# A two-layer gated network on one core: the fifth pass of the first product as pairs of 64-row matmuls

## The chip, the cores and the metric

The kernel runs on one NeuronCore of a Trainium2 chip. The metric is the device time of one execution in microseconds (us), lower is better. The time before is 1227.66 us, the median of three runs that lie between 1227.56 and 1228.3 us.

## The reference, cut to what matters

```python
# x: (2, 4096, 192), weight: (8 heads, 7 taps)
w   = softmax(weight, axis=-1)
out = causal 7-tap convolution of x along the sequence, one set of taps per head
x   = out.reshape(8192, 192)
h   = x @ moe_w_in                     # 192 -> 2048
x   = (h * clip(h + 3, 0, 6) / 6) @ moe_w_out      # 2048 -> 192
h   = x @ moe2_w_in                    # 192 -> 2048
g   = where(h > 0, h, exp(min(h, 0)) - 1)
out = g @ moe2_w_out                   # 2048 -> 192
```

All data are float32.

## The kernel before, in words

**Tiles.** The 8192 tokens are cut into 16 tiles of 512. A tile lies transposed, features on the partitions, 512 tokens along the free axis. The 192 features are split into part a (128 partitions) and part b (64 partitions). The 2048 hidden features are 16 chunks of 128. Two chunks make a group (`CPG` = 2), so a layer of a tile has eight groups (`GROUPS`), and the whole run has 16 x 2 x 8 = 256 groups.

**Precision.** TensorE works in float32r. To keep accuracy each operand is split into a high part (rounded to float32r) and a low part (the rest), and hi x hi, lo x hi and hi x lo are summed in PSUM.

**First product.** `chunk_product` computes a chunk of h. Five matmuls, each of 128 rows by 128 columns of weights and 512 moving columns, accumulate into one PSUM bank: for part a `win_hi_a` x `in_hi_a`, `win_lo_a` x `in_hi_a`, `win_hi_a` x `in_lo_a`; for part b `win_hi_b` x `in_b` and `win_lo_b` x `in_b`. `in_b` holds the high part of the 64 features of b in partitions 0 to 63 and their low part in 64 to 127; the `win_*_b` tiles hold the 64 rows of b twice. So the fourth matmul gives hi x hi and hi x lo in one pass. The fifth gives lo x hi, the wanted term, and lo x lo, which isn't needed. `first_product` does this for the two chunks of a group and adds 1 to `h_ready`.

**Second product.** `second_product` takes the gated values of a group (`g_hi`, `g_lo`) through ten matmuls of the same shape into the accumulators `acc_a` and `acc_b`.

**Order on TensorE.** `phase` is one layer of one tile: for each group g the first product of g and then the second product of g - 2 (`LAG` = 2); the two before that belong to the phase ahead. So TensorE's program is ten matmuls of a first product, ten of a second, in turn, 5120 in all. `pair` orders the phases: layer 1 of tile i, then layer 2 of tile i - 1.

**PSUM.** Eight banks: `h_ps[0]` and `h_ps[1]`, two banks each, by the parity of the group; two for `acc_a` and two for `acc_b`. The first product of group G may begin when group G - 2 has been read (`g_ready` at least G - 1).

**Other engines.** After `h_ready` ScalarE reads `h_ps` into `hidden` (L274 relu for layer 1, L276 exp for layer 2), VectorE combines it with `h_ps` (L404, or L407 and L409) and adds to `g_ready`, ScalarE makes `g_hi` (L284), VectorE `g_lo` (L413). Between these VectorE computes the convolution of a later tile (L355, L357). The input of the next layer is made in `take_mlp1` and `take_mlp1_b`, that of layer 1 in `split_conv`: ScalarE writes the high part (L246, L247, L254, L259), VectorE the low part (L374, L376, L383, L389). GpSimd makes low weights in the first stretch alone; SyncE issues the loads and stores.

Of the kernel before, what the change touches and what calls it, by code (L numbers as in the profile page):

```python
# [29 lines left out]
F32R = mybir.dt.float32r  # L30
# [7 lines left out]
P = 128  # L38
DA = P
DB = D - P  # L40
TOK = 512
# [3 lines left out]
CPG = 2  # L45
# [3 lines left out]
PIECES = 4  # L49
# [3 lines left out]
SIXTH = 1.0 / 6.0  # L53


def build(nc, x_win, tap_w, w_in1, w_out1, w_in2, w_out2, out_t):
    w_in, w_out = (w_in1, w_in2), (w_out1, w_out2)
    with ExitStack() as ctx:
        def sb(name, shape, dt=F32):
            return ctx.enter_context(nc.sbuf_tensor(name, shape, dt))  # L60

        def ps(name, shape):
            return ctx.enter_context(nc.psum_tensor(name, shape, F32))

        def sem(name):
            return ctx.enter_context(nc.semaphore(name))
# [4 lines left out]
        win_hi_b = [sb(f"win_hi_b{m}", [P, FF], F32R) for m in range(2)]  # L71
        win_lo_b = [sb(f"win_lo_b{m}", [P, FF], F32R) for m in range(2)]
# [10 lines left out]
        conv_b = sb("conv_b", [DB, TOK])  # L83
# [4 lines left out]
        in_hi_a = [sb(f"in_hi_a{m}", [DA, TOK], F32R) for m in range(2)]  # L88
        in_lo_a = [sb(f"in_lo_a{m}", [DA, TOK], F32R) for m in range(2)]
        in_b = [sb(f"in_b{m}", [2 * DB, TOK], F32R) for m in range(2)]  # L90

        hidden = sb("hidden", [P, 2, CPG * TOK])
        g_hi = sb("g_hi", [P, PARTS, CPG * TOK], F32R)
# [3 lines left out]
        sum_b1 = sb("sum_b1", [DB, TOK])  # L97
# [5 lines left out]
        h_ps = [ps(f"h_ps{s}", [P, CPG * TOK]) for s in range(2)]  # L103
# [8 lines left out]
        w_split = sem("w_split")  # L112
# [4 lines left out]
        conv_hi = sem("conv_hi")  # L117
        in1_ready = sem("in1_ready")
        in2_ready = sem("in2_ready")
        h_ready = sem("h_ready")  # L120
        act_done = sem("act_done")
        expm1_done = sem("expm1_done")
        g_ready = sem("g_ready")
# [3 lines left out]
        take1 = sem("take1")  # L127
# [16 lines left out]
        def end1(i):  # L144


            return GROUPS if isinstance(i, int) and i == 0 else first_group1(i) + GROUPS
# [88 lines left out]
        def _(act):  # L236
# [5 lines left out]
            def split_conv(t, dst, reused):  # L242
                act.wait_ge(tap_done, 2 * TAPS * t + 2 * TAPS)
                if reused:
                    act.wait_ge(h_ready, end1(t - 1))
                nc.scalar.copy(in_hi_a[dst][:, :], conv_a[:, :]).then_inc(conv_hi, 1)  # L246
                nc.scalar.copy(in_b[dst][0:DB, :], conv_b[:, :]).then_inc(conv_hi, 1)  # L247

            def take_mlp1(t, acc, dst, input_read):

                act.wait_ge(parts_used, end1(t))
                if input_read is not None:
                    act.wait_ge(h_ready, input_read)
                nc.scalar.mul(in_hi_a[dst][:, :], acc_a[acc][:, :], SIXTH).then_inc(take1, 1)  # L254
                nc.scalar.copy(half_b1[:, :], acc_b[acc][DB:2 * DB, :]).then_inc(take1, 1)

            def take_mlp1_b(t, dst):
                act.wait_ge(take1_b, t + 1)
                nc.scalar.mul(in_b[dst][0:DB, :], sum_b1[:, :], SIXTH).then_inc(take1, 1)  # L259

            def take_mlp2(t, acc):
                act.wait_ge(parts_used, end2(t))
                act.wait_ge(stored, 32 * (t + 1))
                nc.scalar.copy(half_b2[:, :], acc_b[acc][DB:2 * DB, :]).then_inc(take2, 1)
                nc.scalar.copy(out_a[:, :], acc_a[acc][:, :]).then_inc(take2, 1)
# [27 lines left out]
            high_weights(2)  # L293
            act.wait_ge(tap_done, 2 * TAPS)
            nc.scalar.copy(in_b[1][0:DB, :], conv_b[:, :]).then_inc(conv_hi, 1)
            act.wait_ge(three_set, 1)

            for g in range(GROUPS):
                nonlinear(0, 0, g)
                if g == TAPS - 1:  # L300
                    split_conv(1, 0, False)
                high_part(0, g)
                if g + 3 < 2 * PIECES:
                    high_weights(g + 3)
# [45 lines left out]
        def _(dve):  # L350
# [19 lines left out]
                    tap(part, k)  # L370

            def split_conv(t, dst):
                dve.wait_ge(conv_hi, 2 * t + 2)
                nc.vector.tensor_tensor(in_lo_a[dst][:, :], conv_a[:, :], in_hi_a[dst][:, :].bitcast(F32),  # L374
                                        ALU.subtract).then_inc(in1_ready, 1)
                nc.vector.tensor_tensor(in_b[dst][DB:2 * DB, :], conv_b[:, :], in_b[dst][0:DB, :].bitcast(F32),  # L376
                                        ALU.subtract).then_inc(in1_ready, 1)

            def take_mlp1(t, acc, dst):
                dve.wait_ge(take1, 3 * t + 2)  # L380
                nc.vector.tensor_tensor(sum_b1[:, :], acc_b[acc][0:DB, :], half_b1[:, :],
                                        ALU.add).then_inc(take1_b, 1)
                nc.vector.scalar_tensor_tensor(out=in_lo_a[dst][:, :], in0=acc_a[acc][:, :], scalar=SIXTH,  # L383
                                               in1=in_hi_a[dst][:, :].bitcast(F32), op0=ALU.mult,
                                               op1=ALU.subtract).then_inc(in2_ready, 1)

            def take_mlp1_b(t, dst):
                dve.wait_ge(take1, 3 * t + 3)
                nc.vector.scalar_tensor_tensor(out=in_b[dst][DB:2 * DB, :], in0=sum_b1[:, :], scalar=SIXTH,  # L389
                                               in1=in_b[dst][0:DB, :].bitcast(F32), op0=ALU.mult,  # L390
                                               op1=ALU.subtract).then_inc(in2_ready, 1)
# [46 lines left out]
            for part in range(2):  # L438
                for k in range(TAPS):
# [3 lines left out]
                    if part == 1 and k == 1:  # L443
                        dve.wait_ge(conv_hi, 1)
                        nc.vector.tensor_tensor(in_lo_a[1][:, :], conv_a[:, :], in_hi_a[1][:, :].bitcast(F32),  # L445
                                                ALU.subtract).then_inc(in1_ready, 1)
            dve.wait_ge(conv_hi, 2)
            nc.vector.tensor_tensor(in_b[1][DB:2 * DB, :], conv_b[:, :], in_b[1][0:DB, :].bitcast(F32),  # L448
                                    ALU.subtract).then_inc(in1_ready, 1)

            for g in range(GROUPS):
                nonlinear(0, 0, g)
                if g < TAPS - 1:
                    conv_tap(1, g)
                    if g == TAPS - 2:
                        conv_tap(1, TAPS - 1)
                if g == TAPS - 1:
                    split_conv(1, 0)
                low_part(0, g)
# [42 lines left out]

        @block.tensor
        def _(pe):
            def chunk_product(m, g, c, src, a=True, b=True):

                f = slice((g * CPG + c) * P, (g * CPG + c + 1) * P)
                dst = h_ps[g % 2][:, c * TOK:(c + 1) * TOK]
                passes = []
                if a:  # L510
                    passes += [(win_hi_a, in_hi_a), (win_lo_a, in_hi_a), (win_hi_a, in_lo_a)]
                if b:
                    passes += [(win_hi_b, in_b), (win_lo_b, in_b)]
                for n, (w, x) in enumerate(passes):
                    mm = nc.tensor.matmul(dst, w[m][:, f], x[src][:, :], start=(a and n == 0),  # L515
                                          stop=(b and n == len(passes) - 1))
                return mm

            def first_product(m, base, g, src, load=False):

                G = base + g
                if load and g % 2 == 0:
                    pe.wait_ge(w_split, 2 * (2 * PIECES * m + g) + 2)
                if not (isinstance(G, int) and G < 2):
                    pe.wait_ge(g_ready, G - 1)
                for c in range(CPG):
                    mm = chunk_product(m, g, c, src)
                mm.then_inc(h_ready, 1)

            def second_product(m, base, g, acc, load=False):  # L530

# [19 lines left out]
            def first_start():  # L551

                pe.wait_ge(in1_ready, 1)
                pe.wait_ge(w_split, 1)
                for g in range(2):
                    for c in range(CPG):
                        chunk_product(0, g, c, 1, b=False)
                pe.wait_ge(in1_ready, 2)
                pe.wait_ge(w_split, 2)
                for g in range(2):  # L560
                    for c in range(CPG):
                        mm = chunk_product(0, g, c, 1, a=False)
                    mm.then_inc(h_ready, 1)

            def phase(m, base, src, before, acc, ready, acc_free, load=False):


                ready()
                for g in range(GROUPS):
                    if before is not None or g >= 2:  # L570
                        first_product(m, base, g, src, load)
                    if g < LAG:
                        if before is not None:
                            before(GROUPS - LAG + g)
                    else:
                        if g == LAG:
                            acc_free()
                        second_product(m, base, g - LAG, acc, load)
# [68 lines left out]
```

## Time and profile before

| | value |
|---|---|
| median of 3 runs | 1227.66 us (1227.56 to 1228.3) |
| profiled execution, its span | 1227.6 us |
| PE (matmuls) busy | 1205.1 us, 98% |
| PEld (weight loads) busy | 967.4 us, 79% |
| DVE (VectorE) busy | 920.2 us, 75% |
| ACT (ScalarE) busy | 620.2 us, 51% |
| POOL (GpSimd) busy | 53.9 us, 4% |
| mean granted TensorE clock | 0.996 |

The profile lists each instruction of an engine with its start and its duration. Matmuls are pipelined: a record goes from the read of the first column to the modelled end, and the next record begins before it. So the cost of a matmul in a dense stream is the distance from start to start, and its record's length says how long the engine needs to run empty. The only time given for the profiled execution is its span, from the first to the last instruction; it agrees with the median of the runs within 0.1 us, so the two are taken as one.

### The profile page before, as it was taken

What the parts mean: (1) busy time and instruction counts of PE and PEld (TensorE: products, weight loads), DVE (VectorE), ACT (ScalarE), POOL (GpSimd) and SP (SyncE); (2) the same over time, 40 slices, a digit from 0 to 9 for tenths busy, and PEclk for the clock granted to TensorE, in tenths of its full rate; (3) what the DMA queues carried; (4) which work ended last, traced back from release to release, by engine and by line L of the source; (5) the groups of instructions that cost most, each with busy time, mean ns of one, the idle gap of its engine ahead of it and who ended that gap; (6) DMA issues with size and microseconds to landing.
All of it is one profiled execution on the core that took longest, in us unless ns stands there. A gap on an engine that the chain in (4) does not pass through costs nothing.

```text
span 1227.6 us, 13953 instructions
## 1 busy us (share of the span) xinstructions
PE 1205.1 (98%) x5120; PEld 967.4 (79%) x5120; DVE 920.2 (75%) x969; ACT 620.2 (51%) x658; POOL 53.9 (4%) x36
## 2 busy tenths in 40 slices
PE   4999999999999999999999999999999999999998
PEld 2888888888888888888888888888888888888886
DVE  7888786877777777777777867778687777776665
ACT  3674555545555454554545545455544555545444
POOL 3472000000000000000000000000000000000000
PEclk8999999999999999999999999999999999999999
DMA  4220000000000000000000000000000000000000
GB/s 133 86 61 14 1 26 0 0 26 0 26 0 21 4 0 26 0 26 0 0 26 0 26 0 0 26 0 26 0 0 26 0 26 0 9 5 5 9 1 26
DMA packets 13727, 20.21 MB, mean 16 GB/s; under 512 B 1424, under 2 KB 5520, under 8 KB 13712
## 3 DMA queue, kind: packets, MB, share of 16 engines
q1 hardware_dynamic: 13568, 20.00, 5.3%
q8 instruction: 10, 0.16, 0.1%
q14 instruction: 5, 0.04, 0.0%
q10 hardware_dynamic: 144, 0.01, 0.0%
HBM read 13.71 MB, written 6.29 MB: 16 GB/s over the span
## 4 chain that ended last, share of the span: by engine, by line
PE 98%; DVE 1%; DMA 0%; ACT 0%; issue 0%; SPq 0%; DVEq 0%; ACTq 0%
PE h_ps L515 49%; PE acc_b L548 10%; PE acc_b L541 10%; PE acc_a L547 10%; PE acc_a L539 10%; PE acc_a L540 10%; DVE conv_b L357 1%; DVE conv_a L357 0%; DMA xwin_b<-x_win 0%; DVE conv_b L355 0%; DVE hidden L404 0%; DVE in_lo_a L445 0%; ACT hidden L274 0%; DVE in_b L448 0%; DVE out_b L396 0%
## 5 line engine op out<-in xcount | busy, mean ns | idle before, releaser
L284 ACT CAST g_hi<-hidden 128x1024 fp32r<-128x1024 f32 x256 | 269.2, 1051 | 371.6 <-DVE hidden L409 244.4
L413 DVE TENSOR_TENSOR g_lo<-hidden,g_hi 128x1024 fp32r<-128x1024 f32 x256 | 313.2, 1223 | 128.0 <-ACT g_hi L284 127.5
L404 DVE SCALAR_TENSOR_TENSOR hidden<-hidden,h_ps 128x1024 f32<-128x1024 f32 x128 | 156.2, 1221 | 111.3 <-ACT hidden L274 111.2
L515 PE MATMUL h_ps<-in_hi_a,win_hi_a 128*128 128x512 f32 x512 | 204.7, 400 | 16.5 <-DVE in_lo_a L445 15.4
L274 ACT ACTIVATE hidden<-h_ps,three 128x1024 f32<-128x1024 f32 x128 | 142.9, 1117 | 131.9 <-PE h_ps L515 131.9
L515 PE MATMUL h_ps<-in_b,win_hi_b 128*128 128x512 f32 x512 | 203.8, 398 | 1.8 <-DVE in_b L448 1.8
L515 PE MATMUL h_ps<-in_hi_a,win_lo_a 128*128 128x512 f32 x512 | 204.4, 399 | 0.0
L515 PE MATMUL h_ps<-in_lo_a,win_hi_a 128*128 128x512 f32 x512 | 204.2, 399 | 0.0
L515 PE MATMUL h_ps<-in_b,win_lo_b 128*128 128x512 f32 x512 | 203.8, 398 | 0.0
L541 PE MATMUL acc_b<-g_hi,wout_b 128*128 128x512 f32 x512 | 203.0, 396 | 0.0
L548 PE MATMUL acc_b<-g_lo,wout_b 128*128 128x512 f32 x512 | 203.0, 396 | 0.0
L547 PE MATMUL acc_a<-g_lo,wout_hi_a 128*128 128x512 f32 x512 | 203.0, 396 | 0.0
L539 PE MATMUL acc_a<-g_hi,wout_hi_a 128*128 128x512 f32 x512 | 203.0, 396 | 0.0
L540 PE MATMUL acc_a<-g_hi,wout_lo_a 128*128 128x512 f32 x512 | 203.0, 396 | 0.0
L276 ACT ACTIVATE hidden<-h_ps 128x1024 f32<-128x1024 f32 x128 | 131.7, 1029 | 80.8 <-PE h_ps L515 80.8
L409 DVE TENSOR_TENSOR hidden<-hidden,h_ps 128x1024 f32<-128x1024 f32 x128 | 156.3, 1221 | 4.4
L515 PEld LDWEIGHTS h_ps<-in_hi_a,win_hi_a 128*128 128x128 f32 x512 | 97.2, 190 | 40.8 <-DVE in_lo_a L445 15.4
L407 DVE TENSOR_SCALAR hidden<-hidden 128x1024 f32<-128x1024 f32 x128 | 89.9, 703 | 52.5 <-ACT hidden L276 51.3
L515 PEld LDWEIGHTS h_ps<-in_b,win_hi_b 128*128 128x128 f32 x512 | 96.8, 189 | 25.9 <-DVE in_b L448 2.3
L515 PEld LDWEIGHTS h_ps<-in_lo_a,win_hi_a 128*128 128x128 f32 x512 | 97.3, 190 | 23.8
L515 PEld LDWEIGHTS h_ps<-in_hi_a,win_lo_a 128*128 128x128 f32 x512 | 97.3, 190 | 23.6
L515 PEld LDWEIGHTS h_ps<-in_b,win_lo_b 128*128 128x128 f32 x512 | 96.9, 189 | 23.6
(47 smaller groups left out, 857.8 us busy)
## 6 DMA issues: line engine op xcount, KB each, us to landing
xwin_a<-x_win SPq DMA_DIRECT2D x16, 259.0 KB, 2.8
raw_in<-w_in SPq DMA_DIRECT2D x8, 512.0 KB, 4.7
out_t<-out_a SPq DMA_DIRECT2D x16, 256.0 KB, 2.6
raw_out<-w_out SPq DMA_DIRECT2D x8, 384.0 KB, 3.6
xwin_b<-x_win SPq DMA_DIRECT2D x16, 129.5 KB, 3.0
out_t<-out_b SPq DMA_DIRECT2D x16, 128.0 KB, 2.3
taps<-tap_w ACTq DMA_DIRECT2D x1, 7.0 KB, 2.3
```

Of the source, the lines that this page charges most:

```text
L274: ins = nc.scalar.activation(hidden[:, g % 2, :], h_ps[g % 2][:, :], ACT.Relu, bias=three[:, 0:1])
L276: ins = nc.scalar.activation(hidden[:, g % 2, :], h_ps[g % 2][:, :], ACT.Exp)
L284: nc.scalar.copy(g_hi[:, g % PARTS, :], hidden[:, g % 2, :]).then_inc(hi_ready, 1)
L404: nc.vector.scalar_tensor_tensor(out=v, in0=v, scalar=6.0, in1=h_ps[g % 2][:, :], op0=ALU.min, op1=ALU.mult).then_inc(g_ready, 1)
L409: nc.vector.tensor_tensor(v, v, h_ps[g % 2][:, :], ALU.max).then_inc(g_ready, 1)
L413: nc.vector.tensor_tensor(g_lo[:, g % PARTS, :], hidden[:, g % 2, :], g_hi[:, g % PARTS, :].bitcast(F32), ALU.subtract).then_inc(lo_ready, 1)
L515: mm = nc.tensor.matmul(dst, w[m][:, f], x[src][:, :], start=(a and n == 0), stop=(b and n == len(passes) - 1))
L539: nc.tensor.matmul(acc_a[acc][:, :], wout_hi_a[m][:, f, :], x, start=first, stop=False)
L540: nc.tensor.matmul(acc_a[acc][:, :], wout_lo_a[m][:, f, :], x, start=False, stop=False)
L541: nc.tensor.matmul(acc_b[acc][:, :], wout_b[m][:, f, :], x, start=first, stop=False)
L547: nc.tensor.matmul(acc_a[acc][:, :], wout_hi_a[m][:, f, :], x, start=False, stop=end)
L548: mm = nc.tensor.matmul(acc_b[acc][:, :], wout_b[m][:, f, :], x, start=False, stop=end)
```

## The change

The fifth matmul of each chunk (`win_lo_b` x `in_b`, 128 rows) is taken out. In its place stands a matmul of 64 rows that computes only lo x hi. For the first chunk of a group it uses partitions 0 to 63, the upper half of the array, for the second chunk partitions 64 to 127, the lower half. The lower half needs the high part of b on partitions 64 to 127, so a second input tile `in_b2` gets it there, by one more ScalarE instruction in each place where `in_b` is written.

The four halves of two successive groups are issued together, in the even group's `first_product`: eight full matmuls of group g, its two halves (they end the sum of group g), the wait for the banks of group g + 1, and the two halves of g + 1 (they begin its sum). In the odd group's `first_product` eight full matmuls remain, and no wait. `first_start` does the same at the very beginning, with both groups' halves at the end. The counts that VectorE waits for (`conv_hi`, `take1`) rise, since each is now added to once more.

```diff
+        in_b2 = [sb(f"in_b2{m}", [2 * DB, TOK], F32R) for m in range(2)]
...
                 nc.scalar.copy(in_b[dst][0:DB, :], conv_b[:, :]).then_inc(conv_hi, 1)
+                nc.scalar.copy(in_b2[dst][DB:2 * DB, :], conv_b[:, :]).then_inc(conv_hi, 1)
...
                 nc.scalar.mul(in_b[dst][0:DB, :], sum_b1[:, :], SIXTH).then_inc(take1, 1)
+                nc.scalar.mul(in_b2[dst][DB:2 * DB, :], sum_b1[:, :], SIXTH).then_inc(take1, 1)
...
             nc.scalar.copy(in_b[1][0:DB, :], conv_b[:, :]).then_inc(conv_hi, 1)
+            nc.scalar.copy(in_b2[1][DB:2 * DB, :], conv_b[:, :]).then_inc(conv_hi, 1)
...
-                dve.wait_ge(conv_hi, 2 * t + 2)
+                dve.wait_ge(conv_hi, 3 * t + 3)
...
-                dve.wait_ge(take1, 3 * t + 3)
+                dve.wait_ge(take1, 4 * t + 4)
...
-                    passes += [(win_hi_b, in_b), (win_lo_b, in_b)]
+                    passes += [(win_hi_b, in_b)]
                 for n, (w, x) in enumerate(passes):
-                    mm = nc.tensor.matmul(dst, w[m][:, f], x[src][:, :], start=(a and n == 0),
-                                          stop=(b and n == len(passes) - 1))
+                    mm = nc.tensor.matmul(dst, w[m][:, f], x[src][:, :], start=(first and n == 0),
+                                          stop=(last and n == len(passes) - 1))
                 return mm
...
+            def half_products(m, g, src, first):
+
+                for c in range(CPG):
+                    rows = slice(c * DB, (c + 1) * DB)
+                    f = slice((g * CPG + c) * P, (g * CPG + c + 1) * P)
+                    mm = nc.tensor.matmul(h_ps[g % 2][:, c * TOK:(c + 1) * TOK], win_lo_b[m][rows, f],
+                                          (in_b, in_b2)[c][src][rows, :], start=first, stop=not first)
+                return mm
+
+            def bank_free(G):
                 if not (isinstance(G, int) and G < 2):
                     pe.wait_ge(g_ready, G - 1)
-                for c in range(CPG):
-                    mm = chunk_product(m, g, c, src)
-                mm.then_inc(h_ready, 1)
+
+            def first_product(m, base, g, src, load=False):
+
+                G = base + g
+                if g % 2 == 0:
+                    if load:
+                        pe.wait_ge(w_split, 2 * (2 * PIECES * m + g) + 2)
+                    bank_free(G)
+                    for c in range(CPG):
+                        chunk_product(m, g, c, src)
+                    half_products(m, g, src, False).then_inc(h_ready, 1)
+                    bank_free(G + 1)
+                    half_products(m, g + 1, src, True)
+                else:
+                    for c in range(CPG):
+                        mm = chunk_product(m, g, c, src, first=False, last=True)
+                    mm.then_inc(h_ready, 1)
...
                 for g in range(2):
                     for c in range(CPG):
-                        mm = chunk_product(0, g, c, 1, a=False)
-                    mm.then_inc(h_ready, 1)
+                        chunk_product(0, g, c, 1, a=False, first=False)
+                for g in range(2):
+                    half_products(0, g, 1, False).then_inc(h_ready, 1)
```

## Rows read from the trace of the kernel before

**Rows 1.** The page: busy time of each engine; the chain that ended last.

```profile
PE 1205.1 (98%) x5120; PEld 967.4 (79%) x5120; DVE 920.2 (75%) x969; ACT 620.2 (51%) x658; POOL 53.9 (4%) x36
...
PE 98%; DVE 1%; DMA 0%; ACT 0%; issue 0%; SPq 0%; DVEq 0%; ACTq 0%
```

**Rows 2.** Waits, whole run: who waited for whom, total us, times, longest.

```profile
PE h_ps L515 <- DVE in_lo_a L445: 15.4, 1, 15.4
...
PE h_ps L515 <- DVE in_b L448: 1.8, 1, 1.8
...
PE h_ps L515 <- DVE hidden L404: 1.1, 1, 1.1
```

**Rows 3.** One tile's length in the middle: busy time, count, granted clock.

```profile
300.00:375.00 75.00, 75.00 (x322) 60.30 (x321) 56.63 (x61) 37.77 (x39) 0.00 (x0) 1.00 0.04 11
```

**Rows 4.** Timeline, layer 1: end of one first product, start of the next.

```profile
602.07 0.39 PE L515 MATMUL h_ps<-in_b,win_lo_b 128*128 128x512 f32 x1
602.07 0.19 PEld L539 LDWEIGHTS acc_a<-g_hi,wout_hi_a 128*128 128x128 f32 x1
602.30 0.40 PE L539 MATMUL acc_a<-g_hi,wout_hi_a 128*128 128x512 f32 x1
...
602.50 1.12 ACT L274 ACTIVATE hidden<-h_ps,three 128x1024 f32<-128x1024 f32 x1 [1.23 <-PE h_ps L515]
...
603.65 1.22 DVE L404 SCALAR_TENSOR_TENSOR hidden<-hidden,h_ps 128x1024 f32<-128x1024 f32 x1 [1.01 <-ACT hidden L274]
...
604.64 0.40 PE L515 MATMUL h_ps<-in_hi_a,win_hi_a 128*128 128x512 f32 x1
```

**Rows 5.** Timeline of PE at the start: a restart from empty, full clock.

```profile
22.46 0.50 PE L515 MATMUL h_ps<-in_b,win_hi_b 128*128 128x512 f32 x1 [1.77 <-DVE in_b L448]
22.80 0.40 PE L515 MATMUL h_ps<-in_b,win_lo_b 128*128 128x512 f32 x1
```

**Rows 6.** Timeline of PEld at the same restart: the two weight loads.

```profile
22.46 0.19 PEld L515 LDWEIGHTS h_ps<-in_b,win_hi_b 128*128 128x128 f32 x1 [2.31 <-DVE in_b L448]
22.57 0.19 PEld L515 LDWEIGHTS h_ps<-in_b,win_lo_b 128*128 128x128 f32 x1
```

**Rows 7.** Timeline, layer 2: PE, and VectorE's reading of the bank.

```profile
564.58 0.40 PE L515 MATMUL h_ps<-in_b,win_lo_b 128*128 128x512 f32 x1
...
569.27 0.39 PE L515 MATMUL h_ps<-in_b,win_lo_b 128*128 128x512 f32 x1
...
566.80 1.22 DVE L409 TENSOR_TENSOR hidden<-hidden,h_ps 128x1024 f32<-128x1024 f32 x1
```

**Rows 8.** Groups of instructions, whole run: busy us, mean ns of one.

```profile
L276 ACT ACTIVATE hidden<-h_ps 128x1024 f32<-128x1024 f32 x128 | 131.7, 1029 | 80.8 <-PE h_ps L515 80.8
L407 DVE TENSOR_SCALAR hidden<-hidden 128x1024 f32<-128x1024 f32 x128 | 89.9, 703 | 52.5 <-ACT hidden L276 51.3
L259 ACT ACTIVATE in_b<-sum_b 64x512 fp32r<-64x512 f32 x16 | 9.9, 616 | 0.0
L247 ACT CAST in_b<-conv_b 64x512 fp32r<-64x512 f32 x15 | 9.3, 617 | 0.0
```

**Rows 9.** Timelines of ACT, PE and DVE in the first 31 us.

```profile
21.07 0.62 ACT L295 CAST in_b<-conv_b 64x512 fp32r<-64x512 f32 x1 [8.26 <-DVE conv_b L357]
...
23.27 0.39 PE L515 MATMUL h_ps<-in_b,win_lo_b 128*128 128x512 f32 x1
...
24.91 1.22 DVE L404 SCALAR_TENSOR_TENSOR hidden<-hidden,h_ps 128x1024 f32<-128x1024 f32 x1 [2.51 <-ACT hidden L274]
...
26.28 0.76 PE L515 MATMUL h_ps<-in_hi_a,win_hi_a 128*128 128x512 f32 x1 [1.11 <-DVE hidden L404]
26.84 0.63 PE L515 MATMUL h_ps<-in_hi_a,win_lo_a 128*128 128x512 f32 x1
...
30.25 0.56 PE L515 MATMUL h_ps<-in_b,win_lo_b 128*128 128x512 f32 x1
...
29.09 1.22 DVE L404 SCALAR_TENSOR_TENSOR hidden<-hidden,h_ps 128x1024 f32<-128x1024 f32 x1 [0.62 <-ACT hidden L274]
```

More of the change, by code:

```diff
@@ L379, in take_mlp1 @@
             def take_mlp1(t, acc, dst):
-                dve.wait_ge(take1, 3 * t + 2)
+                dve.wait_ge(take1, 4 * t + 2)
                 nc.vector.tensor_tensor(sum_b1[:, :], acc_b[acc][0:DB, :], half_b1[:, :],
@@ L446, in _ @@
                                                 ALU.subtract).then_inc(in1_ready, 1)
-            dve.wait_ge(conv_hi, 2)
+            dve.wait_ge(conv_hi, 3)
             nc.vector.tensor_tensor(in_b[1][DB:2 * DB, :], conv_b[:, :], in_b[1][0:DB, :].bitcast(F32),
@@ L504, in _, with chunk_product @@
         def _(pe):
-            def chunk_product(m, g, c, src, a=True, b=True):
+            def chunk_product(m, g, c, src, a=True, b=True, first=True, last=False):
                 f = slice((g * CPG + c) * P, (g * CPG + c + 1) * P)
@@ L512, in chunk_product @@
                 if b:
-                    passes += [(win_hi_b, in_b), (win_lo_b, in_b)]
+                    passes += [(win_hi_b, in_b)]
                 for n, (w, x) in enumerate(passes):
-                    mm = nc.tensor.matmul(dst, w[m][:, f], x[src][:, :], start=(a and n == 0),
-                                          stop=(b and n == len(passes) - 1))
-                return mm
+                    mm = nc.tensor.matmul(dst, w[m][:, f], x[src][:, :], start=(first and n == 0),
+                                          stop=(last and n == len(passes) - 1))
+                return mm
+            def half_products(m, g, src, first):
[6 more added lines that the diff above has]
+            def bank_free(G):
+                if not (isinstance(G, int) and G < 2):
+                    pe.wait_ge(g_ready, G - 1)
             def first_product(m, base, g, src, load=False):
                 G = base + g
[L522 to L525, printed above, removed]
-                for c in range(CPG):
-                    mm = chunk_product(m, g, c, src)
-                mm.then_inc(h_ready, 1)
+                if g % 2 == 0:
[11 more added lines that the diff above has]
+                    mm.then_inc(h_ready, 1)
             def second_product(m, base, g, acc, load=False):
```

## The prediction

> **What bounds the kernel now.** I read the busy times and the chain first: TensorE's matmuls are busy for 1205.1 of 1227.6 us, and 98% of the chain that ended last lies on PE [rows 1]. The table of waits says the same from the other side. PE waited for another engine three times in the whole run, 15.4, 1.8 and 1.1 us, all in the first 27 us [rows 2]. A stretch of 75 us from the middle is filled to the end at a granted clock of 1.00 [rows 3]. So everywhere but in the first 27 us the time is the number of places in TensorE's stream times the length of a place.
>
> A place is the distance from start to start. From 602.07 to 604.64 there are eleven places, 2.57 / 11 = 0.234 us [rows 4]. The last matmuls of two successive first products stand twenty places apart, 564.58 and 569.27, which gives 4.69 / 20 = 0.234 [rows 7]. I use 0.234. A record is 0.40 long, so a matmul is on its way for about 0.16 us more after its successor has started. The reader is to see two things there: the weight load of the next matmul begins when the current one begins (both at 602.07 [rows 4]), so it is covered; and the change from the first product to the second, or from bank to bank, costs nothing.
>
> VectorE, with 56.63 of 75 us, and ScalarE, with 37.77, have room [rows 3].
>
> **What is saved if all goes well.** 256 groups are 128 pairs of groups. A pair had four fifth passes, four places. It now has four halves; if the two of a group run beside each other they need two places. That is 2 x 0.234 = 0.468 us per pair, 128 x 0.468 = 59.9 us in all. The number of instructions doesn't change (5120 matmuls, 5120 weight loads); all of the gain hangs on the overlap.
>
> **What the change of height costs.** The stream was uniform: every matmul uses all 128 rows. Now it changes twice per pair, full to half and back, 256 times in all. No row shows a matmul of 64 rows or such a change, so its price has to be bounded.
>
> Lower bound: nothing. The weights of the half load while the last full matmul runs, as they do today, and the change costs 0.
>
> Upper bound: the array has to be empty before weights can go into it in another division. Then three things stand in a row: the last matmul runs out, 0.397 us from its start (0.40 in the record, 0.396 as the mean of one; ScalarE, which reads its bank, starts 0.43 after it, 602.07 to 602.50, so the record's length is about right [rows 4]); the load; the next matmul. The price of a load that nothing covers is in the restart at 22.46: the first load starts at 22.46 and the second at 22.57; the matmul behind starts at 22.80, 0.34 after the first instead of 0.234, so 0.107 us are open [rows 5, 6]. A change then takes 0.397 + 0.107 = 0.504 from start to start instead of 0.234, an extra 0.270 us.
>
> Which value? The nearest row is the restart from empty, the only place at full clock where a load isn't ahead. The load that runs ahead in the stream today goes into an array that is divided as the running matmul is; for a load that divides it otherwise, I have no row that shows it can be ahead. I take the upper one, without great confidence, and keep 0 for the range.
>
> The Trainium skill's TensorEngine Tiling page (Key Properties) states that changing the tiling mode, as opposed to the tile, drains the TensorE. No row before shows it. By it the sum is the one that I take; without it, the sum would be that of the rival with free changes.
>
> **The block, in order.** Time 0 is the start of the last full matmul. It has run out at 0.397. The load of the upper half ends at 0.504, and its matmul starts; the load of the lower half follows at 0.611, and its matmul starts beside the first. The second upper half is one place behind the first, 0.738. The second lower half starts at 0.611 + 0.234 = 0.845. It has run out at 1.242, and the next full matmul starts after its load at 1.349. Before, the same two full matmuls stood five places apart, 1.171. So a pair becomes 0.178 us longer: 128 x 0.178 = 22.8 us slower. Break-even is near: if the array counts as empty 0.308 us after a start, instead of 0.397, the block costs what it did.
>
> **The wait moved ahead.** The halves of g + 1 write the banks of group g - 1, so `g_ready` of g - 1 is asked for ten places earlier than before, behind the first set of halves. In layer 2, the slower, group g - 1 ends at 564.58 and VectorE has read it at 566.80 + 1.22 = 568.02. The tenth matmul of the next first product, about where the wait will stand, starts at 569.27 [rows 7]. That leaves 1.25 us. In layer 1 VectorE ends at 603.65 + 1.22 = 604.87 and the tenth place is at 604.64 + 9 x 0.234 = 606.75, 1.88 us later [rows 4]. So it is met and I cost it at nothing. If it were late, the second product behind it would be late with it, and all other engines.
>
> **The added ScalarE work.** One more instruction of 0.616 us per write of `in_b`, 32 in all [rows 8]. In `take_mlp1_b` two of them (1.23) stand beside VectorE's L404 of 1.22 us [rows 4]; VectorE waits for them after it. In `split_conv` three stand behind the exp, about 1.85, beside L407 and L409 (0.703 + 1.22 = 1.92), which `high_part` waits for anyway [rows 4, 8]. Both are covered to within 0.1 us, and that is inside the 1.25 us above. Were the cover gone, 0.62 once per layer of a tile would make at most 32 x 0.62 = 20 us, but only after the 1.25 us are used up. GpSimd, SyncE and every DMA keep their work and their order.
>
> **The start.** There PE does wait. The added copy stands behind L295 (21.07, 0.62 long) and ahead of VectorE's last low part: about 0.52 us later, since such copies overlap by a tenth [rows 9]. `h_ready` of group 0 came with the matmul at 23.27; now it comes with the lower half, 0.397 + 0.107 + 0.107 = 0.61 behind the same place. The chain to 26.28, where PE waits for L404, gets 1.1 us longer [rows 9]. Behind it the moved wait bites once: L404 of group 1 ends at 29.09 + 1.22 = 30.31, and the tenth matmul starts at 30.25 [rows 9]. I add 0.4 for it: 1.5 us in all.
>
> **Sum.** 1227.6 + 22.8 + 1.5 = 1251.9, so 1252 us. The span and the median of the runs are the same within 0.1 us.
>
> **The rivals.**
>
> Changes free or nearly so (the other side). The mechanism is one: weights of the other height load ahead, under the running matmul. Then a pair saves 0.468, or 0.361 if the lower half stays behind by its load of 0.107. 1227.6 - 59.9 + 1.5 = 1169, or 1227.6 - 46.2 + 1.5 = 1183 us. For it: all of today's loads are ahead, whatever tile they feed, and nothing in a row says height matters. It decides from the point where a change costs less than 0.18 us (half of 0.361).
>
> The load open, but the next one able to stream in without waiting for the tail. Then the 0.397 in the block becomes 0.234: the block is 0.234 + 0.107 + 0.341 + 0.234 + 0.107 = 1.023 instead of 1.171, 128 x 0.148 = 18.9 us saved, 1210 us. For it: today a new matmul starts 0.16 us before the last has run out. The emptying and the load need not both be exposed.
>
> The halves don't overlap, so that the change doesn't do what it says. Then four halves take four places. With free changes nothing is won: 1229 us. With emptying: 0.397 + 0.107 + 3 x 0.234 + 0.397 + 0.107 = 1.710, 0.539 more per pair, 1227.6 + 69.0 + 1.5 = 1298 us. Against it: the two halves share no rows, no bank and no input tile. The Trainium skill's page TensorE: Matmul & The Clock Gate (Part 3, Measured speedup vs the span model) gives 3.07 times for four row tiles of 32 rows, so it has them overlap. No row before shows this.
>
> TensorE's clock. It fell once in the run, behind idle times of 1 us and more [rows 2, 9]; there a place was 0.43 (26.84 after a first one at 26.28 that had an open load). The new gaps are 0.27 us. A fall for a tenth of the run would cost about 100 us; I give it almost nothing.
>
> **How the numbers follow.** Emptying at each change, halves side by side: 0.46, forecast 1252, own range 1242 (emptying in 0.36) to 1261 (0.43). Open load without emptying: 0.22, near 1210. Free changes: 0.16, 1169 to 1183. No overlap with emptying: 0.07, 1298. No overlap, free changes: 0.05, 1229. The remaining 0.04 is spread above. The range 1176 to 1264 leaves out the lower half of the free case, the 1298 and the tails. Within 0.2% of before, 2.5 us, is about what a measurement here can tell from no change. The case at 1229 and the crossings of the 0.22 and 0.46 cases near break-even give 0.07. Faster: 0.40. Slower: 0.53.
>
> **What the profile after would show.** The last full matmul to the first upper half: 0.50 by my forecast, 0.34 by the open load, 0.234 if free. The same back to full height. Upper to lower half 0.107, against 0.234 if they don't overlap. PE's waits still only in the first 30 us. VectorE's and ScalarE's idle times larger. I am wrong if weight loads of the new height start together with the last full matmul.

## The result, and the profile after

The changed kernel takes 1222.6 us (median of 4 runs, 1222.41 to 1223.79) against 1227.7 us before; the ratio is 0.9961 with a 95% interval of 0.9949 to 0.9972. It is faster by 0.4%, 5.1 us. The forecast was 1252 us, slower by 2%.

Ahead of the prediction the span of the profiled execution before (1227.6 us) and the median of the runs were taken as one. They aren't: every run that has both shows a device time 1.8 us longer than its span. So the profiled execution before is about 1.8 us slower than the median run, at a mean granted clock of 0.996, where nineteen later runs of that kernel have 0.998 to 1.000. Below, spans are set beside spans and medians beside medians.

The page of the changed kernel, busy times and the chain that ended last, answers to [rows 1]:

```profile
PE 1196.2 (98%) x5120; PEld 899.4 (74%) x5120; DVE 918.1 (75%) x969; ACT 640.5 (52%) x690; POOL 52.4 (4%) x36
...
PE 97%; DVE 2%; ACT 0%; DMA 0%; issue 0%; ACTq 0%
PE h_ps L519 39%; PE acc_a L562 12%; PE acc_b L564 10%; PE acc_a L570 10%; PE acc_b L571 10%; PE acc_a L563 10%; PE h_ps L528 7%; DVE conv_a L361 1%; DVE conv_b L361 0%; DVE hidden L408 0%; DMA taps<-tap_w 0%; ACT hidden L277 0%; DVE in_lo_a L449 0%; DVE conv_b L359 0%; ACT g_hi L287 0%
```

TensorE is still the bound, with the same 5120 matmuls. L528 is the new half product. One group of L528 shows the engine at work; this is the timeline of PE in layer 1, where [rows 4] stood before:

```profile
600.89 0.40 PE L519 MATMUL h_ps<-in_b,win_hi_b 128*128 128x512 f32 x1
601.22 0.74 PE L528 MATMUL h_ps<-in_b,win_lo_b 64*128 64x512 f32 x4
601.89 0.50 PE L562 MATMUL acc_a<-g_hi,wout_hi_a 128*128 128x512 f32 x1
602.23 0.40 PE L563 MATMUL acc_a<-g_hi,wout_lo_a 128*128 128x512 f32 x1
```

And the weight loads of the same stretch:

```profile
600.66 0.19 PEld L519 LDWEIGHTS h_ps<-in_b,win_hi_b 128*128 128x128 f32 x1
601.22 0.30 PEld L528 LDWEIGHTS h_ps<-in_b,win_lo_b 64*128 64x128 f32 x4 [0.37 <-issue]
601.89 0.19 PEld L562 LDWEIGHTS acc_a<-g_hi,wout_hi_a 128*128 128x128 f32 x1 [0.37 <-issue]
602.00 0.19 PEld L563 LDWEIGHTS acc_a<-g_hi,wout_lo_a 128*128 128x128 f32 x1
```

Four things are to be seen.

- The first load of a half comes 0.33 us behind the start of the last full matmul (600.89 to 601.22). In the stream a load starts with the matmul ahead of it. So the change of height does make the engine wait, and 0.33 is longer than a place (0.234) and shorter than a matmul's record (0.40). In this block it is 0.326; over all blocks after the first 45 us it is 0.318 to 0.327, on average 0.322.
- Four loads of 0.19 us each fit into 0.30 us: two start together (0.004 us apart in the trace), and two more 0.11 behind them. The lower half's load does not queue behind that of the upper half.
- The four halves end 0.74 after 601.22, at 601.96. The last of them are 0.39 long, so the second pair starts at 601.57, one place and one load (0.34) behind the first.
- From 601.57 to 601.89 the engine empties again (0.32), and L562 has an open load: 0.50 long instead of 0.40, and its successor comes after 0.34 us.

The block, from the last full matmul to the place where the next one streams, is 0.326 + 0.107 + 0.234 + 0.326 + 0.107 = 1.100 us here, on average 1.097. Five places were 1.171. The stream as a whole says the same: the 4640 matmuls behind the 200th (116 pairs of groups) take 1087.08 us before and 1078.41 after, 0.075 us less per pair.

The waits answer to [rows 2] (who waited for whom, total us, times, longest):

```profile
PEld h_ps L528 <- issue: 47.8, 128, 0.7
...
PEld acc_a L562 <- issue: 46.4, 126, 0.4
...
PE h_ps L519 <- DVE in_lo_a L449: 16.2, 1, 16.2
...
PE h_ps L519 <- DVE hidden L408: 2.2, 1, 2.2
PE h_ps L519 <- DVE in_b L452: 2.2, 1, 2.2
...
PE h_ps L528 <- DVE hidden L408: 0.8, 1, 0.8
```

The two "issue" rows are new, one for each direction of the change, once in (nearly) every block. "Issue" means that the load waited for nothing that the profile shows, no other engine and no DMA. The moved wait shows once (0.8 us, at the start), and nowhere else.

The start lost more than forecast. Timeline of PE in the changed kernel, first 40 us:

```profile
16.22 0.80 PE L519 MATMUL h_ps<-in_hi_a,win_hi_a 128*128 128x512 f32 x1 [16.22 <-DVE in_lo_a L449]
...
25.00 1.22 PE L528 MATMUL h_ps<-in_b,win_lo_b 64*128 64x512 f32 x4
28.41 0.47 PE L519 MATMUL h_ps<-in_hi_a,win_hi_a 128*128 128x512 f32 x1 [2.20 <-DVE hidden L408]
...
32.50 0.80 PE L528 MATMUL h_ps<-in_b,win_lo_b 64*128 64x512 f32 x2 [0.84 <-DVE hidden L408]
33.23 0.80 PE L562 MATMUL acc_a<-g_hi,wout_hi_a 128*128 128x512 f32 x1
33.82 0.63 PE L563 MATMUL acc_a<-g_hi,wout_lo_a 128*128 128x512 f32 x1
...
39.12 0.40 PE L562 MATMUL acc_a<-g_hi,wout_hi_a 128*128 128x512 f32 x1
```

The same matmul as the last of these, in the kernel before:

```profile
35.34 0.39 PE L539 MATMUL acc_a<-g_hi,wout_hi_a 128*128 128x512 f32 x1
```

It is 3.8 us later. 0.8 of that is there already at the first matmul (15.38 before); nothing of the change lies ahead of it, and in the traces of the ten kernels shown here that matmul stands anywhere between 15.17 and 17.47. The other 3.0 us are the later `h_ready` of group 0, the wait of 0.84 at 32.50, and the clock: behind idle time the engine ran at the lower of its two levels (1.2 and 2.4 GHz), where the record at 33.82 is 0.63 long instead of 0.40. The kernel before had such a stretch too, of about 7 us against about 10 us here. At that level a place is 0.43 instead of 0.234 us, so the 3 us more cost at most about 1.5 us, by my estimate; no run takes the clock and the later signals apart.

The account closes: 128 x 0.075 = 9.6 us saved, 3.8 us lost, 5.8 us. The two spans, 1227.6 and 1222.0, differ by 5.6, the medians by 5.1.

### The profile page after: what moved, and what is told of

The parts are those of the page before. It is cut to its first block, busy times and chain, and to the rows that moved or that the text cites. A ratio compares the mean times of both kernels' runs of the same rounds, so it can differ in the third digit from the quotient of the medians.

```text
span 1222.0 us, 13985 instructions
## 1 busy us (share of the span) xinstructions
PE 1196.2 (98%) x5120; PEld 899.4 (74%) x5120; DVE 918.1 (75%) x969; ACT 640.5 (52%) x690; POOL 52.4 (4%) x36
## 4 chain that ended last, share of the span: by engine, by line
PE 97%; DVE 2%; ACT 0%; DMA 0%; issue 0%; ACTq 0%
PE h_ps L519 39%; PE acc_a L562 12%; PE acc_b L564 10%; PE acc_a L570 10%; PE acc_b L571 10%; PE acc_a L563 10%; PE h_ps L528 7%; DVE conv_a L361 1%; DVE conv_b L361 0%; DVE hidden L408 0%; DMA taps<-tap_w 0%; ACT hidden L277 0%; DVE in_lo_a L449 0%; DVE conv_b L359 0%; ACT g_hi L287 0%
## 5 line engine op out<-in xcount | busy, mean ns | idle before, releaser
L562 PE MATMUL acc_a<-g_hi,wout_hi_a 128*128 128x512 f32 x512 | 216.5, 423 | 0.0
L562 PEld LDWEIGHTS acc_a<-g_hi,wout_hi_a 128*128 128x128 f32 x512 | 96.6, 189 | 64.6 <-issue 46.4
L571 PEld LDWEIGHTS acc_b<-g_lo,wout_b 128*128 128x128 f32 x512 | 96.5, 189 | 23.6
```

What stands on the lines that cost most here:

```text
L562: nc.tensor.matmul(acc_a[acc][:, :], wout_hi_a[m][:, f, :], x, start=first, stop=False)
L571: mm = nc.tensor.matmul(acc_b[acc][:, :], wout_b[m][:, f, :], x, start=False, stop=end)
```

## The experiments

**All halves in the upper half of the array**

```diff
-                    rows = slice(c * DB, (c + 1) * DB)
+                    rows = slice(0, DB)
...
-                                          (in_b, in_b2)[c][src][rows, :], start=first, stop=not first)
+                                          in_b[src][rows, :], start=first, stop=not first)
```

> All four halves use partitions 0 to 63 (in_b), so no two can run beside each other; the changes of height stay. Theory A (the two halves of a group overlap fully, each change of height waits until the array has run out, 0.326 us from the last start, and then 0.107 for an open load): the block, from the last full matmul to the next full one, goes from 1.100 to 0.326 + 0.107 + 3 x 0.234 + 0.326 + 0.107 = 1.568 us; 128 x 0.468 = 59.9 more than the 1222.6 of the changed kernel, about 1282 us. Theory B (halves did not overlap, and the gain came from somewhere else, such as shorter records): no change, about 1222 us.

Measured: 1279.78 us, ratio 1.0421 (1.0404 to 1.0439). Timeline of PE:

```profile
607.73 0.39 PE L519 MATMUL h_ps<-in_b,win_hi_b 128*128 128x512 f32 x1
608.05 1.19 PE L528 MATMUL h_ps<-in_b,win_lo_b 64*128 64x512 f32 x4
609.17 0.50 PE L562 MATMUL acc_a<-g_hi,wout_hi_a 128*128 128x512 f32 x1
609.51 0.40 PE L563 MATMUL acc_a<-g_hi,wout_lo_a 128*128 128x512 f32 x1
```

The four take 1.19 us instead of 0.74, two places more; the gaps on both sides stay (607.73 to 608.05, and an open load in L562). The overlap of upper and lower half is real and is worth 57.2 us here. Within one height the next load is ahead again, since the added halves cost a place each and no load. All four read `in_b` here and the gaps stay, so the reading of the second tile `in_b2` doesn't make them.

**Full matmuls in the same places**

```diff
-                    rows = slice(c * DB, (c + 1) * DB)
...
-                    mm = nc.tensor.matmul(h_ps[g % 2][:, c * TOK:(c + 1) * TOK], win_lo_b[m][rows, f],
-                                          (in_b, in_b2)[c][src][rows, :], start=first, stop=not first)
+                    mm = nc.tensor.matmul(h_ps[g % 2][:, c * TOK:(c + 1) * TOK], win_lo_b[m][:, f],
+                                          in_b[src][:, :], start=first, stop=not first)
```

> The new order, the moved wait and the added ScalarE copies stay, but the four matmuls of the block are full ones of 128 rows (lo x lo included, as in the kernel before). Theory A (the gaps of 0.326 come from the change of height): they disappear, the block is five places, 1.171 us, and the time is 1222.6 + 128 x 0.071 = 1231.7, less up to 1 us of the start: 1230 to 1232 us. Theory C (the gaps come from the wait placed in the block, the added read of a second tile or the semaphore in the middle): they stay, the block is 1.100 + 0.468 = 1.568, about 1282 us.

Measured: 1231.77 us, ratio 1.0034 (1.0023 to 1.0046). Timeline of PE:

```profile
603.93 0.40 PE L519 MATMUL h_ps<-in_b,win_hi_b 128*128 128x512 f32 x1
604.17 1.09 PE L527 MATMUL h_ps<-in_b,win_lo_b 128*128 128x512 f32 x4
605.10 0.39 PE L561 MATMUL acc_a<-g_hi,wout_hi_a 128*128 128x512 f32 x1
```

No gap: 603.93 to 605.10 is five places. Order, moved wait, semaphores and ScalarE's extra copies are all still in, so none of them makes the gap; the change of height does. Those other parts cost 4 us against the kernel before, all of it in the start: behind the 200th matmul the two streams take the same time, 1087.08 us for the next 4640 matmuls.

**One group at a time**

```diff
-                if g % 2 == 0:
-                    if load:
...
-                    half_products(m, g, src, False).then_inc(h_ready, 1)
-                    bank_free(G + 1)
-                    half_products(m, g + 1, src, True)
-                else:
...
+                bank_free(G)
+                for c in range(CPG):
+                    chunk_product(m, g, c, src)
+                half_products(m, g, src, False).then_inc(h_ready, 1)
```

> The halves are issued group by group, two at a time, behind each group's eight full matmuls; 512 changes of height instead of 256, and the wait for the banks is where it was before the change. Theory A: a group's block is 0.326 + 0.107 + 0.326 + 0.107 = 0.866 us instead of three places, 0.703; two groups cost 1.732 against 1.100 + 0.234 = 1.334 in the changed kernel, 128 x 0.398 = 50.9 more, about 1273 us. Theory D (the cost of the change of height is small and most of the missing gain is in the moved wait): at or below 1222 us.

Measured: 1268.27 us, ratio 1.0328 (1.0311 to 1.0346). Timeline of PE:

```profile
600.67 0.39 PE L519 MATMUL h_ps<-in_b,win_hi_b 128*128 128x512 f32 x1
600.99 0.49 PE L528 MATMUL h_ps<-in_b,win_lo_b 64*128 64x512 f32 x2
601.42 0.50 PE L555 MATMUL acc_a<-g_hi,wout_hi_a 128*128 128x512 f32 x1
601.75 0.40 PE L556 MATMUL acc_a<-g_hi,wout_lo_a 128*128 128x512 f32 x1
```

From 600.67 to 601.42 plus a load of 0.107 is 0.86 us (0.850 on average), close to the expected 0.866 and more than the three places (0.703) that it replaces. The run is 5 us under the expectation; with the averages of the blocks, 1.700 for two groups against 1.331, nearly 4 of them are explained. Two changes of height for one saved place lose; two changes for two saved places just win.

**The four halves crossed**

```diff
-                    half_products(m, g, src, False).then_inc(h_ready, 1)
+                    half_product(m, g, 0, src, False)
                     bank_free(G + 1)
-                    half_products(m, g + 1, src, True)
+                    half_product(m, g + 1, 0, src, True)
+                    half_product(m, g, 1, src, False).then_inc(h_ready, 1)
+                    half_product(m, g + 1, 1, src, True)
...
```

`half_product` issues one of the two matmuls of `half_products`.

> The same four halves in another order: upper g, upper g+1, lower g, lower g+1. Theory A with matmuls that start in program order: the second upper half waits a place for the first, the first lower half starts beside it, the second lower half a place later. Three places instead of two: 128 x 0.234 = 30 more, about 1252 us. Rival: the engine pairs whatever is free, then 1222 us. If two upper halves in a row break the overlap altogether, four places and 1282 us.

Measured: 1222.66 us, ratio 0.9953 (0.9937 to 0.9970). My expectation of 1252 failed; the rival's 1222 came. Timelines of PE and of ACT:

```profile
600.80 0.40 PE L519 MATMUL h_ps<-in_b,win_hi_b 128*128 128x512 f32 x1
601.13 0.74 PE L532 MATMUL h_ps<-in_b,win_lo_b 64*128 64x512 f32 x4
601.79 0.50 PE L567 MATMUL acc_a<-g_hi,wout_hi_a 128*128 128x512 f32 x1
```

```profile
601.91 1.11 ACT L277 ACTIVATE hidden<-h_ps,three 128x1024 f32<-128x1024 f32 x1 [1.44 <-PE h_ps L532]
```

ACT in the changed kernel, for comparison:

```profile
601.77 1.11 ACT L277 ACTIVATE hidden<-h_ps,three 128x1024 f32<-128x1024 f32 x1 [1.20 <-PE h_ps L528]
```

The four again take 0.74, so they run in two places, and two upper halves can't share one (the first experiment). So the lower half of g, third in the program, ran beside the upper half of g, ahead of the upper half of g + 1. The trace shows it directly: of the four records the one that adds to `h_ready`, the lower half of g, is the second to start, 0.007 us behind the first, in every block after the first 45 us. Its result is signalled later, though: ScalarE starts 0.78 us behind the start of the four, 0.55 in the changed kernel (601.22 to 601.77), one place more. The semaphore itself says the same: `h_ready` rises 0.755 us behind that start, on average, and 0.521 in the changed kernel. That fits starts that are free between the halves of the array and completions that are reported in program order, behind the upper half of g + 1.

**The lower half left out**

```diff
-                for c in range(CPG):
+                for c in range(1):
                     rows = slice(c * DB, (c + 1) * DB)
...
-                        mm = chunk_product(m, g, c, src, first=False, last=True)
+                        mm = chunk_product(m, g, c, src, first=(c == 1), last=True)
```

> Leaves out the lower half of the array: lo x hi of part b is not added for the second chunk of each group. 256 matmuls fewer. Theory A (the lower half runs fully beside the upper one, and its weights load beside those of the upper one): the block stays at 1.100 us, 1222.6 us. If the partner costs anything in streaming or loading, each 0.01 us of it shows as 256 x 0.01 = 2.6 us less.

Measured: 1220.07 us (1219.16 to 1221.36), ratio 0.9940 (0.9926 to 0.9953). Timeline of PE:

```profile
606.44 0.39 PE L519 MATMUL h_ps<-in_b,win_hi_b 128*128 128x512 f32 x1
606.76 0.73 PE L528 MATMUL h_ps<-in_b,win_lo_b 64*128 64x512 f32 x2
607.42 0.50 PE L562 MATMUL acc_a<-g_hi,wout_hi_a 128*128 128x512 f32 x1
```

The block without partners is 606.44 to 607.42, 0.98 us and its load; with them it was 1.00 and its load. On average the difference, with the load, is 0.011 us per block, 1.4 of the 2.5 us; the rest isn't placed, and the two intervals overlap.

**The start, three ways.** First, the whole first phase as before:

```diff
             nc.scalar.copy(in_b[1][0:DB, :], conv_b[:, :]).then_inc(conv_hi, 1)
-            nc.scalar.copy(in_b2[1][DB:2 * DB, :], conv_b[:, :]).then_inc(conv_hi, 1)
...
+                if isinstance(base, int) and base == 0:
+                    if g % 2 == 0:
+                        pe.wait_ge(w_split, 2 * g + 2)
+                    bank_free(G)
+                    for c in range(CPG):
+                        chunk_product(m, g, c, src)
+                        mm = full_low(m, g, c, src)
+                    mm.then_inc(h_ready, 1)
+                elif g % 2 == 0:
...
```

`full_low` is the fifth pass of the kernel before, with all 128 rows.

> The whole first phase (layer 1 of tile 0, eight groups) runs as in the kernel before: full fifth passes, no moved wait, no copy to in_b2 at the start. Theory S (the start lost 3.8 us by the 40th matmul: in the trace 36.78 against 32.99): that loss goes, and of the four blocks of this phase 4 x 0.071 = 0.3 us of gain go too: 1222.6 - 3.8 + 0.3 = 1219.1 us. Rival (the late start was the run's own, from loads and a slower VectorE instruction): 1222 us.

Measured: 1218.73 us (1218.45 to 1218.99), ratio 0.9926 (0.9912 to 0.9939). Its interval lies wholly below that of the changed kernel, and it beats both. The matmul that stood at 35.34 before and at 39.12 after the change is here:

```profile
33.84 0.40 PE L574 MATMUL acc_a<-g_hi,wout_hi_a 128*128 128x512 f32 x1
```

It is 1.5 us earlier than before the change, although up to there the two programs on TensorE are the same and the first matmul stands 1.4 us later (16.75). What differs is the clock. These are the stretches from 20 to 40 us of the kernel before, the changed kernel and this one (the granted clock is the third number from the end):

```profile
20.00:40.00 20.00, 17.12 (x61) 12.81 (x60) 14.97 (x18) 11.70 (x16) 8.49 (x6) 0.83 0.43 138
20.00:40.00 20.00, 14.78 (x46) 9.54 (x45) 12.54 (x15) 10.89 (x15) 6.95 (x5) 0.74 0.44 135
20.00:40.00 20.00, 17.38 (x71) 13.37 (x70) 14.96 (x17) 11.25 (x15) 8.47 (x6) 1.00 0.45 138
```

The mean granted clock is 0.999 to 1.000 in the five runs here and 0.995 to 0.998 in the four of the changed kernel. So Theory S gave the right number, but what the old start gives back is in part a clock that doesn't fall, and no run shows how large that part is.

Second, only groups 0 and 1 as before, with the copy to `in_b2` off VectorE's way:

```diff
-            dve.wait_ge(conv_hi, 3)
+            dve.wait_ge(conv_hi, 2)
...
                 for g in range(2):
                     for c in range(CPG):
                         chunk_product(0, g, c, 1, a=False, first=False)
-                for g in range(2):
-                    half_products(0, g, 1, False).then_inc(h_ready, 1)
+                        mm = full_low(0, g, c, 1)
+                    mm.then_inc(h_ready, 1)
+                pe.wait_ge(conv_hi, 3)
```

> Only groups 0 and 1 run as in the kernel before, and the copy to in_b2 is off VectorE's way; groups 2 to 7 of the first phase keep the blocks and the moved wait. Theory S1 (most of the lost 3.8 us comes from the late h_ready of group 0 and the copy): near 1220 us. Theory S2 (it comes from the moved wait of group 3): 1221.5 to 1222.6 us.

Measured: 1221.19 us (1219.66 to 1221.33), ratio 0.9944 (0.9931 to 0.9958). It lies between the two theories, and its interval overlaps that of the changed kernel: the runs don't split the loss between `h_ready` and the moved wait.

Third, the copy alone off VectorE's way:

```diff
-            dve.wait_ge(conv_hi, 3)
+            dve.wait_ge(conv_hi, 2)
...
+                pe.wait_ge(conv_hi, 3)
                 for g in range(2):
                     half_products(0, g, 1, False).then_inc(h_ready, 1)
```

> The changed kernel, but at the start VectorE no longer waits for the copy to in_b2; TensorE does, ahead of the first halves. By the profile's 0.5 us of such a copy: 1222.6 - 0.5 = 1222.1 us; if the copy wasn't on the path: 1222.6 us.

Measured: 1221.73 us (1221.28 to 1223.12), ratio 0.9951 (0.9937 to 0.9964). The expected half microsecond is less than the runs can tell.

## Why the prediction was wrong, point by point

**What bounds the kernel** was right: TensorE, whose time is places plus gaps.

**What is saved**, 0.468 us per pair from the overlap, 59.9 us in all, was right. Take it away, and 57.2 us come back.

**What the change of height costs.** The kind of cost was right: a wait ahead of the load, and then an open load. It stands once in each direction in every block, and it is gone in the run with full matmuls. The load was right too, 0.107. The Trainium skill's TensorEngine Tiling page (Key Properties) says that a change of tiling mode drains the TensorE; the traces agree, with 0.32 us from the start of the last matmul to the load. That this time is an emptying and not some fixed time of the change isn't shown: all matmuls here have 512 columns, and no run varied that.

**The block, in order** is the step that failed, by the size of two terms.

- The emptying. I took the record's length, 0.397 us. It took 0.322 on average, at both ends: 2 x 0.075 = 0.150 us per block. ScalarE's start 0.43 behind the last matmul seemed to support 0.397, but it tells when the results can be read and not when the next load may begin.
- The stagger. I had the lower half's load wait for the upper one's, 0.107 us, and carried that to the end of the block, with no row that showed it. They go in together, 0.004 us apart.

Together 0.252 us per block, 1.349 - 1.097, and 128 x 0.252 = 32.3 us. Break-even was stated at an emptying of 0.308 with the stagger in. Without the stagger it is at 0.308 + 0.107 / 2 = 0.362, and 0.322 is on the winning side of it. With the measured emptying and the stagger kept, the block is 1.199, still slower than 1.171; so it took both terms to turn the sign.

**The wait moved ahead** and **the added ScalarE work** were right for the body: PE waited for VectorE at a half product only once, 0.8 us, in the start.

**The start** was forecast at 1.5 us and came out at 3.8 in the profile. What the forecast left out is the longer stretch at the lower clock there, and 0.8 us that were late before the first matmul and aren't the change's. The clock stayed at 1.00 behind the start, so the forecast was right that the new gaps don't lower it.

With the measured terms the sum is 1251.9 - 32.3 + 2.3 = 1221.9 us; measured 1222.6.

**The rivals.** None came as described. By its number the nearest is the one without overlap and with free changes, 1229 us, and both of its parts are excluded: the overlap is there and the changes cost. The one with an open load and no emptying, 1210 us, is 13 us away on the other side. I had given "faster" 0.40; the weight on one row for the emptying, near a break-even that I had worked out myself, was too large.

## What to carry to other kernels

- A pair of half-height matmuls saves one place (0.234 us here), but each stretch of them costs two changes of height, each 0.322 + 0.107 - 0.234 = 0.2 us. Count places saved per stretch: one loses (one_group, 1268 us), two win a little (1222.6 us), and every further pair in the same stretch should be worth a whole place, an estimate from these rows that no run tried.
- Try the old form where the bound engine waits for others anyway. Here that was the first phase, and it gave 3.9 of the 8.9 us that the best version gains, part of it through a clock that didn't fall.
- When a forecast hangs on a term that is within a quarter of its break-even, the sign is open, whatever row the term is taken from.

## What the runs showed of the hardware

- Ahead of a change of height the next weight load starts 0.32 us (0.318 to 0.327) behind the start of the last 512-column matmul at full clock, 0.07 less than its record is long. It was the same in both directions and in all kernels whose last matmul had its own weights loaded ahead; in the run with one group at a time the last half has an open load itself, and it is 0.42.
- Weights for the upper and the lower half of the array load at the same time: two loads of 0.19 us started 0.004 us apart, and four stood within 0.30 us.
- Matmuls of different halves of the array need not start in program order (the crossed halves ran in two places, not three, and the third in the program started 0.007 us behind the first), while the semaphore of the one that ran early came a place later (0.755 instead of 0.521 us behind the start of the four). The Trainium skill's page TensorE: Matmul & The Clock Gate (Part 3, The mechanism) has matmuls start and end in program order. This trace agrees for the end and not for the start, and the measurement decides.
